# Aligned tensors, other routing groups and later tables in a fused attention and expert kernel

## The reference

```python
def _attn_ref(q, k, v):                # 2 x 8 heads x 768 x 64
    ...                                # window of 16 each way, plus 24 block summaries
    return np.matmul(a, v_all).astype(np.float32)

def _moe_ref(x, w_gate, w_noise, noise, w1, w2):   # x: 1536 x 512, 8 experts, 1024 wide
    noisy_logits = x @ w_gate + np.log1p(np.exp(x @ w_noise)) * noise
    top2 = np.argpartition(-noisy_logits, 2, axis=1)[:, :2]
    ...
    for e in range(E):
        for k in range(2):
            mask = top2[:, k] == e
            h = np.maximum(x[mask] @ w1[e], 0.0)
            out[mask] += top2_w[mask, k, None] * (h @ w2[e])

def _moe2_ref(x, w_in, w_out, s, b):   # 512 -> 2048 -> 512
    r = np.maximum(x @ w_in, 0.0)
    return (s * (r * r) + b) @ w_out
```

## Time and profile before

| what | value |
|---|---|
| median of three runs | 742.96 us (742.82 to 743.03) |
| the profiled execution | 744.61 us |
| its span, first to last instruction | 742.9 us |
| PE busy | 700.6 us (94%) |
| PE weight loads busy | 574.1 us (77%) |
| POOL, DVE, ACT busy | 315.5, 263.1, 215.4 us |
| mean granted clock of PE | 0.968 |

### The profile page before, as it was taken

How to read it: one execution, slowest core, us unless ns; L and a number is a source line. 1 busy time by engine, 2 the same in 40 slices (tenths; PEclk the granted TensorE clock), 3 DMA queues, 4 the chain that set the end, 5 groups by cost and what they waited for, 6 DMA issues and landing times.

```text
span 742.9 us, 10458 instructions
## 1 busy us (share of the span) xinstructions
PE 700.6 (94%) x4065; PEld 574.1 (77%) x4065; DVE 263.1 (35%) x550; ACT 215.4 (29%) x499; POOL 315.5 (42%) x286
## 2 busy tenths in 40 slices
PE   7798779899999897999899999999999999999995
PEld 3466568788888686787789898888888888888883
DVE  5367547531231313211121225746505235052220
ACT  2457845221220211212112212312314113242121
POOL 1325614578987296298879751502021020200002
PEclk9999958999999999899999999999999999999998
DMA  9987432599979196394698798952012020100001
GB/s 253 230 242 208 157 115 86 189 389 377 396 249 384 43 352 208 103 393 131 225 348 291 249 305 326 349 180 57 1 47 66 1 56 1 57 0 1 1 0 56
DMA packets 56350, 132.37 MB, mean 178 GB/s; under 512 B 9352, under 2 KB 11656, under 8 KB 56304
## 3 DMA queue, kind: packets, MB, share of 16 engines
q0 software_dynamic: 28592, 83.83, 33.2%
q1 hardware_dynamic: 27091, 46.74, 20.5%
q10 hardware_dynamic: 621, 1.18, 0.7%
HBM read 104.81 MB, written 25.99 MB: 176 GB/s over the span
## 4 chain that ended last, share of the span: by engine, by line
PE 85%; DMA 4%; DVE 4%; ACT 2%; issue 2%; another core or an unknown queue 1%; POOL 1%; SPq 0%; POOLq 0%; ACTq 0%; DVEq 0%
PE ps L369 25%; PE ps L371 25%; PE ps L370 25%; DMA v_all<-in_v_dram 2%; PE ps L1513 2%; PE ps L1429 1%; PE ps L1373 1%; PE ps L1446 1%; PE ps L1409 1%; PE ps L1388 1%; DMA k_sb<-in_kT_dram 1%; ACT prob L676 1%; PE ps L1651 1%; PE ps L1438 1%
## 5 line engine op out<-in xcount | busy, mean ns | idle before, releaser
L530 POOL TENSOR_TENSOR w_lo<-w_raw,w_hi 128x1024 fp32r<-128x1024 f32 x56 | 134.3, 2418 | 24.9 <-DMA w_hi<-in_w_pieces_dram 24.7
L950 DVE SCALAR_TENSOR_TENSOR h_lo<-ps,h_hi 128x448 fp32r<-128x448 f32 (+2 forms) x64 | 36.7, 574 | 213.7 <-ACT h_hi L687 213.7
L369 PE MATMUL ps<-x_hi,w_hi 128*128 128x448 f32 (+2 forms) x256 | 88.6, 346 | 3.4 <-DVE h_lo L950 3.4
L369 PE MATMUL ps<-w_hi,h_hi 128*128 128x512 f32 x216 | 88.9, 411 | 0.0
L371 PE MATMUL ps<-x_hi,w_lo 128*128 128x448 f32 (+2 forms) x256 | 88.3, 345 | 0.0
L370 PE MATMUL ps<-x_lo,w_hi 128*128 128x448 f32 (+2 forms) x256 | 88.1, 344 | 0.0
L370 PE MATMUL ps<-w_lo,h_hi 128*128 128x512 f32 x216 | 86.2, 399 | 0.0
L371 PE MATMUL ps<-w_hi,h_lo 128*128 128x512 f32 x216 | 86.2, 399 | 0.0
L687 ACT ACTIVATE h_hi<-ps 128x448 fp32r<-128x448 f32 (+2 forms) x64 | 32.2, 505 | 181.6 <-PE ps L371 171.0
L1295 DVE SCALAR_TENSOR_TENSOR sqr<-relu,sbb 128x512 f32<-128x512 f32 x48 | 36.1, 753 | 117.1 <-ACT relu L821 116.4
L630 POOL DMA_INDIRECT out_dram<-osb,ord_i x12 | 11.6, 969 | 155.1 <-ACT osb L833 155.1
(11 more groups left out here) (227 smaller groups left out, 1176.8 us busy)
## 6 DMA issues: line engine op xcount, KB each, us to landing
w_raw<-in_w_pieces_dram POOLq DMA_DIRECT2D x56, 512.0 KB, 14.9
w_hi<-in_w_pieces_dram POOLq DMA_DIRECT2D x56, 512.0 KB, 14.4
xb<-x_sorted SPq DMA_DIRECT2D x25, 256.0 KB, 7.5
y_sorted<-ysb SPq DMA_DIRECT2D x25, 256.0 KB
x_sorted<-zrow SPq DMA_DIRECT2D x7, 896.0 KB, 15.3
w_raw<-in_w_pieces_dram SPq DMA_DIRECT2D x8, 512.0 KB, 6.7
w_hi<-in_w_in_dram POOLq DMA_DIRECT2D x8, 512.0 KB, 7.8
w_raw<-in_w_in_dram SPq DMA_DIRECT2D x8, 512.0 KB, 7.7
```

What stands on the lines that cost most here:

```text
L369: pe.matmul(acc, l_hi, r_hi, start=start, stop=False, skip_group_check=True)
L530: pool.tensor_tensor(piece(w_lo, slot, k), piece(w_raw, slot, k), piece(w_hi, slot, k).bitcast(F32), ALU.subtract).then_inc(pieces_split, 1)
L950: dve.scalar_tensor_tensor(out=lo[:, at, i % FT, 0:rows], in0=ps[:, i % FT, 0:rows], scalar=0.0, in1=hi[:, at, i % FT, 0:rows].bitcast(F32 ...
```

## The change

Four things are changed, and no instruction is added or removed except by the sizes of the groups.

- `LARGE = 512`: tensors of 512 bytes a partition or more begin on multiples of 512, and so do the places behind which others are laid by hand. In the program as built, `w_hi`, `w_lo` and `w_raw` move from bytes 16512 and 82048 to 16896 and 82432, `x_hi` from 188352 to 188928, `y_hi` from 171968 to 172544, `x_sb` from 179904 to 181248. 16512 and 82048 are 128 past a multiple of 512; 188352 and 171968 are 64 short of one.
- `GROUP_OF` becomes tiles 0 to 3, 4 to 6, 7 to 9 and 10 to 11; `GMAX` and the place of a count in PSUM follow.
- DVE's `route_a`, `route_top` and `route_chosen`, `route_c` of the first group move from rounds 5, 6 and 7 to 4, 5 and 6, and its `ranks` on PE from round 7 to 6, with the wait for the read of the ranks.
- In `do_head` of DVE, `order_tokens` and `overflow_tables` move behind `turned_head(p + 1)`.

```diff
+LARGE = 512
-GROUP_OF = ((0, 5), (5, 7), (7, 10), (10, 12))
+GROUP_OF = ((0, 4), (4, 7), (7, 10), (10, 12))
-GMAX = 5
+GMAX = 4
-L_HALF = L_RANK + 5 * E
+L_HALF = L_RANK + GMAX * E
-        base = (nc.sbuf_base + 63) // 64 * 64
+        base = (nc.sbuf_base + LARGE - 1) // LARGE * LARGE
             def tensor(self, name, shape, dt):
                 size = int(np.prod(shape[1:])) * (2 if dt == BF16 else 4)
+                unit = LARGE if size >= LARGE else 64
+                self.at = (self.at + unit - 1) // unit * unit
                 t = nc.alloc_sbuf_tensor_at(name, shape, dt, offset=self.at)
-                self.at += (size + 63) // 64 * 64
+                self.at += size
                 return t
+            def rounded(self):
+                self.at = (self.at + LARGE - 1) // LARGE * LARGE
+                return self.at
...
+        top.rounded()
...
+        att.rounded()
...
-                if s in (5, 7, 10):
-                    route_a((5, 7, 10).index(s))
-                if s in (6, 8):
-                    route_top(s // 2 - 3)
-                if s == 7:
+                if s in (4, 7, 10):
+                    route_a(s // 3 - 1)
+                if s in (5, 8):
+                    route_top(s // 3 - 1)
+                if s == 6:
                     route_c(0)
...
-                if s in (6, 8):
-                    route_chosen(s // 2 - 3)
+                if s in (5, 8):
+                    route_chosen(s // 3 - 1)
...
+                if p + 1 < E:
+                    turned_head(p + 1)
+                if p == 1:
+                    gates_out()
                 if p == 2:
                     order_tokens()
                 if p == 3:
                     overflow_tables()
-                if p + 1 < E:
-                    turned_head(p + 1)
-                if p == 1:
-                    gates_out()
...
-                if s == 8:
+                if s == 7:
                     pe.wait_ge(rank_read, 1)
...
-                if s == 7:
+                if s == 6:
                     pe.wait_ge(xT_ready, s)
                     ranks(0)
```

## The result

The changed kernel took 724.5 us in the median of four runs (722.41 to 725.88), beside 743.0 us (742.82 to 747.19) for the kernel before; the ratio is 0.974, with an interval of 0.969 to 0.978. The profiled execution took 723.52 us around a span of 721.8, against the 723.9 around 722.2 that the prediction gave. The median lies 2.2 us above the forecast of 722.3 and inside its range. The sum behind the forecast did not hold, as the profile shows at once.

A forecast was written before the change was run, and what follows sets the result against it. PE was taken to set the end, with 85% of the span, so only its waits or slow running could be won. 10.7 + 10.0 + 0 = 20.7 us took the median from 742.96 to 722.3 us; range 706 to 733.

The forecast's parts named there:

- part 2: Attention: regrouping tiles as 4, 3, 3 and 2 breaks up POOL's ten scatters in a row, ending slow tiles; 10.0 us.
- Part 1: Last blocks of heads 2 and 3: tables moved behind the next head's rows end PE's waits for `x_lo`; 10.7 us.
- The cover: DVE's free time before the next head's `h_lo`, 9.26 us, holds the longer table, 7.07 us, with 2.2 us to spare.
- the pause should let it in: Attention: a 2 us break before POOL's last six scatters lets PE's next block of code arrive before tile 10's scores.
- PE ran out of code, and new code reached it slowly: Attention, 88.4 to 99.3 us: PE's slow score matmuls lacked code while POOL issued indirect DMAs; tiles 9 to 11 lost 10.0 us.
- nothing, if the third run hurts as before: Lower bound for the regrouping in attention: the last six scatters still slow PE; some 2 us won at best.
- Part 3: Tensors on multiples of 512 bytes: matmul pace taken as unchanged, 0 us; up to 2.6 us at the start allowed in range.
- The count of 2,736: Number of three-pass matmuls in the program; 5.0 ns on each would be 13.7 us either way.
- The rival with faster moving weights: Down and out products, 1,272 matmuls, fall from 233.3 to 228.3 ns; 6.4 us more won, 715.9 us; 18%.
- The slower case: Aligned operands collide, every three-pass matmul loses 5.0 ns, 13.7 us, while scatters still slow PE; 746.0 us; 3%.
- The warm-up pace of 216 ns: All 2,736 three-pass matmuls reach the pace of the bf16 warm-up, 14.8 ns less each, 40 us; 682 us; 3%.
- Tables alone at 732.3: Only the moved tables win, 10.7 us; the last six scatters still slow PE's next block of code; 27%.

## Why the prediction was right, and where it was not

The total was right by luck, because wrong terms cancelled; in the spans of the two profiles, of the 10.0 us of part 2 only 1.1 came, and the missing 8.9 were made up by 5.8 from the addresses (4.9 in the dense layer, 0.9 in the heads behind), 2.4 at the start, which is in no part's account, and 1.0 more from the tables.

**Part 1, right.** Forecast 10.7 us from the distances in the earlier trace rows; measured 3.92 and 7.07 us in the two blocks, 11.7 over the whole stretch with the clock that came back behind them, 11.1 with the tables alone on chip B. The cover held, and nothing new waited.

**Part 2, wrong.** I took 10.0 us; the profile has 1.1 in attention on chip A, chip B has 2.0 for the groups alone, and on chip D the new groups cost 4.9 us. Of its reading of the earlier trace rows the half stood up that makes the scatters the cause: holding them moved the stall, spacing them ended it. Two steps failed.

The first is "by then the second run is over, so the pause should let it in". I had inferred from one run of four at the earlier trace rows that short runs are harmless. On chip A after the change, two runs of four each slowed a tile (8.32 and 8.44 us), and the run of six brought the rest. The run of four before the change was not harmless either: the `x_sb` of tile 8 in the earlier trace rows waits 0.78 us for "remote", and the semaphore behind it came 1.9 us after the last values matmul, in place of 0.25. The number in a run does not decide. Beside the 29.7 us of chip B, tiles 7 to 11 lose 13 to 14 us on chips C and D with runs of 4, 4 and 6, 12.8 with fourteen in one run, and 11.5 with 4 and 10.

The second is "PE ran out of code, and new code reached it slowly". The runs show late semaphores instead, 11.5 us in tile 9 of the kernel before, and no block of code at the time when the stall ended. So nothing shows that the block of code behind 88 us was waited for; and the score matmuls beside it are those of tile 11, not 10, since they come behind the values of tile 9. The size was off as well, 13.1 us of slow tiles and not 10.0. The bound at the other end, "nothing, if the third run hurts as before", was nearer the truth, but for a reason that I did not name: the first two hurt as well.

**Part 3, wrong in size.** I took 0 "because all the rows lie within 5 ns of each other", though they all lay 12 to 17 ns above the warm-up. The periods fell from 233.3 and 228.3 ns to 226.7, by 6.6 and 1.6; on the dense layer that is 4.9 us, on the heads about 1. The count of 2,736 was too high for a period taken at 512 columns: the heads' 864 `up` products and 48 of the first chunk's have 448, 384 or 256 columns, and the 448-column ones became slower. The rival with faster moving weights had put down 5.0 ns on 1,272 matmuls, 6.4 us, and 18%: about the right amount, and right on the side of the moving weights, but it blamed one operand where chip C shows that only both together do it. The rule that I had cited beside this (the Trainium skill, SBUF — State Buffer, Door 1) would have left the sum as it was; here 64-byte multiples were not enough for the full pace, and the measurement decides. For the start, the estimate of 1.5 us by the Trainium skill (DMA: Bandwidth & Descriptors, How a descriptor splits into AXI transactions) can be neither confirmed nor denied: the mark spreads by 7.7 us with aligned rows and by 5.3 with unaligned ones. That section of the Trainium skill speaks of bytes fetched, and the addresses that moved here are those that the load writes.

**The rivals.** The slower case needed 7.6 ns more on every matmul with both gains; the periods fell. The warm-up pace of 216 ns was not reached. Tables alone at 732.3 is closest to what part 2 really did, and without the addresses and the start it would have been the result: 742.96 less 11.7 and 1.1 is 730.2.

## What to carry to other kernels

Where PE shows "issue" gaps or half clock beside indirect transfers, look at the engines that wait for PE: a wait with the releaser "remote" in a program on one core, long after the matmul it waits for, is the sign of this stall. Then look at how POOL issues the transfers, and put a short other operation between two: 0.37 us of memset each removed 12.4 us of slow tiles. Check it on more than one chip, for chip B had no such stall. The version that comes out best is the changed kernel with spaced scatters, 720.22 us against 728.66 and 743.17 on chip D (0.968 of the kernel before, 0.960 to 0.975); the old groups with spaced scatters may be better still, and were not tried. And when a layout is rounded to a boundary, round both operands of a matmul: one alone won nothing in the dense layer.

## What the runs showed of the hardware that I had not expected

- The kernel before took 743.0, 744.5 and 743.2 us on chips A, C and D and 729.6 on B; beside the groups-only kernel on chip B, the kernel before on chip A shows 13.7 us more for tiles 7 to 11 and 5.2 more for ACT's late copies ahead of head 5, less 4.8 that the faster chip loses waiting for the first expert's rows.
- With fourteen indirect transfers back to back PE stood still for 11.4 us, at a DMA share of 0.51, because the semaphore of a matmul that started at 93.60 came at 104.34. Why a memset or a wait on POOL between the transfers shortens this is not shown. Blocks of code do come in during such a run: the kernel with the old groups had one at 89.8 us, in the middle of ten scatters, and was slow there all the same.
- One 512-column three-pass matmul costs 226.7 to 233.3 ns, in the mean of a chunk's products, by the addresses of its two operands.
- The start of one and the same program differed by 6.6 us between its profiles on chips A, C and D (31.71 to 38.26 us to the first `x_sb`), about as much as the parts were meant to win. Whether that is the chip or the single execution is not shown.
